# A three-stage attention and mixture kernel: the next expert's weight pieces split two, three, two and one at a time over an expert's first slots

## What is computed

```python
logits = x @ w_gate
e_idx = np.argmax(logits, axis=1)
...
for e in range(E):
    mask = e_idx == e
    ...
    h = np.maximum(x[mask] @ w1[e], 0.0)
    ye = h @ w2[e]
    out[mask] = gate_w[mask, None] * eom[mask, e, None] * ye
```

## Time and profile before

| | |
|---|---|
| median of 3 runs | 1162.81 us (1161.41 to 1162.92) |
| the profiled execution's own time | 1161.72 us |
| its span, first to last instruction | 1160.0 us |
| mean granted TensorE clock | 0.977 |
| busy share of the span | PE 94%, PEld 78%, DVE 51%, ACT 33%, POOL 18% |
| expert stage | from 641.1 us to the end |

### The profile page before, as it was taken

How to read it: one execution, slowest core, us unless ns; L and a number is a source line. 1 busy time by engine, 2 the same in 40 slices (tenths; PEclk the granted TensorE clock), 3 DMA queues, 4 the chain that set the end, 5 groups by cost and what they waited for, 6 DMA issues and landing times.

```text
span 1160.0 us, 22528 instructions
## 1 busy us (share of the span) xinstructions
PE 1086.9 (94%) x6180; PEld 901.1 (78%) x6181; DVE 587.3 (51%) x1217; ACT 380.0 (33%) x644; POOL 204.6 (18%) x375
## 2 busy tenths in 40 slices
PE   5799999999999999999994899999999999999695
PEld 4677888888888888888883688888888888888584
DVE  6765766666675766666664243433333332342420
ACT  3333333333333333333331233423334342332321
POOL 2343110212021110212021111111111111111110
PEclk9899999999999999999997899999999999999898
DMA  8432221222112211222000443442324232142000
GB/s 263 131 119 73 73 56 53 73 72 64 56 62 72 72 63 45 73 72 67 25 20 19 128 138 108 137 134 70 123 81 135 92 114 95 63 131 79 27 29 28
DMA packets 57270, 96.70 MB, mean 83 GB/s; under 512 B 15759, under 2 KB 15887, under 8 KB 57233
## 3 DMA queue, kind: packets, MB, share of 16 engines
q1 hardware_dynamic: 47168, 75.60, 20.1%
q0 software_dynamic: 7968, 20.61, 5.9%
q10 hardware_dynamic: 2096, 0.04, 0.1%
HBM read 76.66 MB, written 20.60 MB: 84 GB/s over the span
## 4 chain that ended last, share of the span: by engine, by line
PE 81%; DVE 10%; issue 4%; ACT 2%; DMA 1%; ACTq 0%; POOL 0%; DVEq 0%; SPq 0%; POOLq 0%
PE Y_ps L425 37%; PE H_ps L425 26%; PE T L417 6%; PE S_ps L469 3%; PE X_ps L479 3%; PE X_ps L417 2%; DVE dl L673 2%; PE S_ps L417 2%; DVE prob L720 1%; DVE prob L701 1%; DVE smax L698 1%; DVE ssum L713 1%; PE L_ps L447 1%; ACT dh L554 1%; DVE wx L673 1%
## 5 line engine op out<-in xcount | busy, mean ns | idle before, releaser
L425 PE MATMUL Y_ps<-wx,dh 128*128 (+1 forms) x1216 | 387.9, 400 | 2.2 <-DVE dl L673 2.0
L425 PE MATMUL H_ps<-wx,xh 128*128 (+1 forms) x1216 | 337.8, 400 | 12.3 <-DVE wx L673 8.7
L425 PEld LDWEIGHTS H_ps<-wx,xh 128*128 128x128 f32 x1216 | 226.1, 191 | 58.0 <-issue 12.1
L425 PEld LDWEIGHTS Y_ps<-wx,dh 128*128 128x128 f32 x1216 | 221.0, 189 | 48.9 <-issue 8.1
L425 PE MATMUL Y_ps<-wx,dl 128*128 (+1 forms) x608 | 238.7, 393 | 0.0
L425 PE MATMUL H_ps<-wx,xl 128*128 (+1 forms) x608 | 189.2, 393 | 0.0
L673 DVE TENSOR_TENSOR wx<-stage,wx (+1 forms) x62 | 75.3, 1225 | 157.8 <-ACT wx L626 156.9
L425 PEld LDWEIGHTS H_ps<-wx,xl 128*128 128x128 f32 x608 | 115.3, 190 | 25.1
L425 PEld LDWEIGHTS Y_ps<-wx,dl 128*128 128x128 f32 x608 | 114.6, 188 | 25.6
L969 POOL TENSOR_TENSOR var<-sumsq,rden 128x1 f32<-128x1 f32 x36 | 6.9, 192 | 425.1 <-ACT stage L604 425.1
L673 DVE TENSOR_TENSOR dl<-X_ps,dh 128x512 fp32r<-128x512 f32 x76 | 52.0, 684 | 53.9 <-ACT dh L554 53.9
(11 more groups left out here) (163 smaller groups left out, 1269.0 us busy)
## 6 DMA issues: line engine op xcount, KB each, us to landing
stage<-in_moe_w SPq DMA_DIRECT2D x128, 256.0 KB, 3.0
stage<-in_q SPq DMA_DIRECT2D x36, 256.0 KB, 2.8
stage<-in_k SPq DMA_DIRECT2D x72, 128.0 KB, 2.9
stage<-in_v SPq DMA_DIRECT2D x36, 256.0 KB, 3.1
x_rows<-x SPq DMA_DIRECT2D x36, 256.0 KB, 2.0
stage<-in_moe_w_in SPq DMA_DIRECT2D x3, 512.0 KB, 8.3
stage<-in_moe_w_out SPq DMA_DIRECT2D x3, 512.0 KB, 4.3
slot_rec<-route_table SPq DMA_DIRECT2D x40, 2.0 KB, 1.6
```

Source lines behind the costliest of these rows:

```text
L425: i = pe.matmul(acc[:, c0:c0 + HALF], x[:, kk, :], w(part, kk * cols + c0), start=first and x is hi and part == 0, stop=last and x is lo)
```

## The change

```diff
-SPLIT_RATE = 2
+SPLIT_RATE = 5
+SPLIT_FIRST = 2
 LOAD_RATE = 2
...
-            link(dve.tensor_scalar(idx, idx, 1.0, float(PIECES), ALU.add, ALU.min))
+            link(dve.tensor_scalar(idx, idx, float(SPLIT_FIRST), float(PIECES), ALU.add, ALU.min))
```

## The result

The changed kernel takes 1219.82 us, the median of four runs (1217.72 to 1224.48), against 1162.79 us: a ratio of 1.050 (95% interval 1.047 to 1.053), 57 us more. The profiled execution has a span of 1219.5 us against 1160.0, and a mean granted clock of 0.954 against 0.977. The first stage is as it was: TensorE is busy for 590.7 us of its first 622, against 591.1.

A forecast was written before the change was run, and what follows sets the result against it. TensorE was taken as always busy from 665 to 1080 us, so every new wait costs its full length. 13.7 + 3 x 9.4 + 3.7 - 3.4 + 8.6 = +50.8 us gave 1214 us, range 1196 to 1229.

The forecast's parts named there:

- What bounds the kernel: Expert stage: TensorE is busy in every microsecond from 665 to 1080 us, so any new wait costs its whole length.
- Part 1: End group of slot 35: six pieces become three, H(36) starts 3.4 us earlier, 5.3 us of waiting and the slow restart stay.
- Part 2: Positions 0 and 1, data present: more split pieces delay dl by 1.14 us each, within the margin; costed at nothing.
- Part 3: Expert 0, slot 1: pieces are split before they land; piece 14 comes late and Y(1) waits 13.7 us.
- Part 4: Load bursts ahead of a record: gathered rows late by 9.4 us three times (five loads), 3.7 us for slot 12 (four).
- Part 5: Clock: slow restarts behind the new pauses, 1.83 us for each of four and 1.3 for the shorter, together 8.6 us.
- A: Rival: SyncE's queue keeps up and only the 3.4 us gain before H(36) is seen, 1159.4 us; chance 0.03.
- B: Rival: only expert 0 waits and the load bursts are hidden, 1175 us; chance 0.09.
- F: Rival: no change, gains and losses cancel; chance 0.01.
- E: Rival: load bursts alone cost time, as piece 14 comes earlier than thought, 1198 us; chance 0.06.
- C: Rival: load bursts go quicker, 4.93 us a turn, each five-load wait 3.3 us shorter; +36.7 us, 1200 us; chance 0.13.
- D: Rival: bursts go slower (6.02 us a turn), records start later or extra splits cost 4 us; up to 1226 us; chance 0.15.

The follow-up runs named there:

- experiment 3: Against the kernel before: splits by the new table from expert 1 on, expert 0 by the old, loads by the table of before; 1161.18 us, 0.9985.
- experiment 4: Against the kernel before: splits unchanged, loads of three slots held back and requested together, five at once in slots 13, 18, 23 and 30; 1209.84 us, 1.041.
- experiment 7: Against the kernel before: only expert 6's splits changed, four in slot 34's end group, three in slot 35's middle and one in its end group; 1157.25 us, 0.9952.
- experiment 8: Against the kernel before: only expert 6's splits changed, five in slot 34's end group, three in slot 35's middle group, none after; 1156.38 us, 0.9951.

## Why the prediction was right, and where it was off

The time of 1220 us lies in the range of 1196 to 1229, 6 us above the forecast of 1214; the mechanism, the places and the signs were those of the forecast. Several of its sizes were off, and some of these errors cancelled.

**What bounds the kernel** held: each wait came through to the end in full, as the account of H's starts shows.

**Part 1** held to a tenth, 3.4 us. That the slow restart of H(36) would stay was right, but it grew: 7.93 us for H(36), where it was 7.29 behind the longer pause.

**Part 2** held from expert 1 on (experiment 3). In slot 1 it missed by 0.5 us: the two pieces of slot 0 let the second dl end at 659.83, and Y(0) started at 660.15, when it could have at 659.7. I had costed this on slot 1's rows alone, and slots 0 and 1 lie closer together than others, as no Y runs between their two H.

**Part 3.** The walk met the rows within 0.8 us at each step. After the change, ScalarE and SyncE:

```profile
665.84 1.06 ACT L627 ACTIVATE wx<-stage  x1 [1.64 <-DMA stage<-in_moe_w]
666.80 0.67 ACT L652 ACTIVATE x<-Y_ps,slot_rec 128x512 f32<-128x512 f32 x1
...
672.44 0.35 SPq L375 DMA_DIRECT2D slot_rec<-route_table  x1
...
675.62 0.35 SPq L385 DMA_DIRECT2D stage<-in_moe_w  x1
...
680.08 1.06 ACT L627 ACTIVATE wx<-stage  x1 [7.81 <-DMA stage<-in_moe_w]
```

Predicted were 665.6, 666.6, 673.2, 676.4 and 680.6, and 685.0 for Y(1), which came at 684.46. The wait was 11.8 us and not 13.7 mainly because TensorE itself reached Y(1) 1.1 us later: 0.5 us by Part 2, and 0.6 because H(0), at the start of the stage, took 8.5 us to the transposes behind it where it had taken 6.9, having begun 0.95 earlier. No moved split stands before H(0), so that part isn't the change's work. This part of the loss had only moved: H(3) is 15.8 us late against 15.5 predicted.

**Part 4** had the right four places and was 1.4, 0.1 and 0.3 us short on the bursts of five, 2.2 on the burst of four. Three terms were off and in part cancelled, which is luck and makes two of these misses look smaller than the errors behind them. In slot 17 the four turns took 21.6 us, not 23.0: only the first is long (6.7), the others are 4.9 to 5.1. I had taken the turn from slots in which every second one has a store or a gather beside it; rows 6 had the nearer value. The record ahead of the burst was issued 6.4 us after H(18), not 5.0; I had picked the shorter of my two rows (5.0 and 6.0). The store that this record waits for took 4.3 us, with a weight load issued half a microsecond behind it; the median of these stores is 2.8. And from the gather to TensorE it was 4.5 us, not 3.33, with a weight load (issued at 922.56) and a scatter (923.61) at the same time.

**Part 5** is the term most mis-sized. I took 1.83 us for each restart behind a long pause from one row. The five new pauses cost 2.9, 2.1, 2.3, 1.3 and 2.1 us on the 24 matmuls, and 0.5 more on the four transposes where these came first: 12.7 us against 8.6.

Together: predicted +50.8 us, measured +59.5 on the profiled execution. Of the 8.7 us between, 4.1 are the restarts (12.7 less 8.6), 3.9 the four waits for rows (35.8 less 31.9) and 0.6 the slower H(36); Part 3 gave 0.8 back, and about 1 us is spread over slots that I can't assign. Of the rivals, A, B and F are contradicted by the result (B by experiment 4 as well: bursts do hold up records), E by the wait in slot 2. C and D were both in part true, a quicker turn with a later start of it. The figure of the Trainium skill ("DMA: Bandwidth & Descriptors", section "Anatomy of one DMA — SWDGE (gpsimd) path") is given there for DMAs that GpSimd issues, and these loads are SyncE's. The estimate from it, a turn 0.4 shorter than 5.75, was nearer for the turn, as slot 17 has 5.4 on the mean, and farther off for the sum.

## What to carry to other kernels

A rate that is set in a table may not be what bounds it: "two requests a slot" had stopped binding by slot 11, and the loads followed the splits, so moving the splits moved the loads. Before work is pulled forward, look at what else is put into motion by it, and at what is queued behind that in order: here a 2 KB record behind five loads that wait for each other. And a remedy for one place (expert 6 with two tiles) belongs there alone: used everywhere the table cost 57 us, used there it gives 0.3%, with better shares 0.5%.

## What the hardware showed that I had not expected

The cost of a pause isn't a function of its length in these runs. H(36) restarted in 7.29 and 7.50 us behind a pause of 8.7 (the kernel before and experiment 4) and in 7.58 to 8.29 behind one of 5.3, in six kernels. And H(0), behind a pause of 16 to 17 us and the same code in all of them, took 7.07 us in the kernel before and 7.76 to 8.39 in seven others. Windows of the changed kernel around the start of H(36) (us, busy times, clock, DMA share, GB/s):

```profile
1144.30:1149.50 5.20, 0.00 (x0) 0.00 (x0) 5.04 (x6) 3.64 (x5) 1.36 (x1) 0.81 0.13 50
1149.50:1153.50 4.00, 3.93 (x9) 3.14 (x10) 0.86 (x2) 0.00 (x0) 0.97 (x1) 0.50 0.12 23
```

The granted clock is 0.81 over the pause, which is 2.4 GHz in most of it and 1.2 GHz in the rest; it is at the lower level (0.50) for the 4.0 us behind the restart. Behind the longer pause of the kernel before it was 0.59 over 4.2 us. A pause of 3.0 us ahead of H(36) cost 0.3 us beyond its own length, with the clock at 1.00 (experiment 7), and one of 2.8 us ahead of Y(34) cost 1.8, with 0.57 over the 4 us from its end (experiment 8). These two kernels differ by where one piece is split. What decides it these runs don't show; I leave it open.
